# Block attention ahead of two mixtures of experts: the scores and values as 64 by 64 products, q and v sent without zeros, and the first layer's dense products in four banks of PSUM

## What is computed

```python
q_c, k_c, v_c = (a.reshape(B, H, nc, 64, D) for a in (q, k, v))  # B 4, H 8, S 576, D 64
scores = scale * np.matmul(q_c, k_c.transpose(0, 1, 2, 4, 3))    # 64 x 64 for each chunk and head
attn = softmax(scores)                                           # max, exp, sum + 1e-9, divide
x = np.matmul(attn, v_c)                                         # -> (2304, 512), all heads side by side
for e in range(4):   out += p[:, e:e+1] * (relu(x @ w1[e]) @ w2[e])        # first mixture, all rows
for e in range(8):   out[mask] = gate[mask] * (relu(x[mask] @ v1[e]) @ v2[e])  # second, rows of expert e
```

## Time and profile before

| | |
|---|---|
| median of 3 runs | 1189.31 us (1189.1 to 1190.2) |
| time of the profiled execution | 1190.13 us |
| its span | 1188.1 us |
| PE busy | 1172.5 us, 99% of the span |
| weight loads (PEld) busy | 1042.7 us, 88% |
| DVE, ACT, POOL busy | 519.3, 264.5, 312.0 us |
| read from memory | 82.92 MB |

### The profile page before, as it was taken

The page is one execution under the profiler, slowest core; times in us unless marked ns, Lnnn a source line. Parts: engine busy times, 40 slices in busy tenths (PEclk is TensorE's granted clock), DMA queues, the critical chain, the costliest instruction groups (busy, mean ns, idle before and its releaser), DMA issues.

```text
span 1188.1 us, 18269 instructions
## 1 busy us (share of the span) xinstructions
PE 1172.5 (99%) x6211; PEld 1042.7 (88%) x6212; DVE 519.3 (44%) x1142; ACT 264.5 (22%) x413; POOL 312.0 (26%) x191
## 2 busy tenths in 40 slices
PE   9999999999999999999999999999999999999995
PEld 7998998999999999999999999999887888888884
DVE  5542442422222223222222228888745654555554
ACT  3221222223111113211111411211144023022230
POOL 6400000006000003300000600000186868077580
PEclk9999999999999999999999999999999999999998
DMA  9313222042000002100000400111382564063530
GB/s 361 110 66 106 73 86 106 18 143 89 1 0 0 0 0 90 52 0 0 0 0 1 140 1 28 27 27 27 64 267 60 156 190 166 0 207 124 186 143 15
DMA packets 51471, 92.91 MB, mean 78 GB/s; under 512 B 8431, under 2 KB 33135, under 8 KB 51314
## 3 DMA queue, kind: packets, MB, share of 16 engines
q1 hardware_dynamic: 46082, 78.63, 20.6%
q0 software_dynamic: 4496, 11.56, 3.3%
q10 hardware_dynamic: 864, 2.36, 0.5%
HBM read 82.92 MB, written 10.92 MB: 79 GB/s over the span
## 4 chain that ended last, share of the span: by engine, by line
PE 92%; DVE 3%; DMA 2%; ACT 1%; issue 1%; SPq 0%; ACTq 0%; DVEq 0%; POOL 0%; POOLq 0%
PE psum L1245 14%; PE psum L1247 14%; PE psum L1246 14%; PE psum L1276 10%; PE psum L1278 10%; PE psum L1277 10%; PE psum L1455 3%; PE psum L1457 3%; PE psum L1456 3%; PE psum L1187 3%; PE psum L1172 2%; PE psum L1439 2%; DMA rows<-x_rows,meta 1%; PE psum L1416 1%; DVE xlo L759 1%
## 5 line engine op out<-in xcount | busy, mean ns | idle before, releaser
L431 POOL TENSOR_TENSOR weights_r<-weights,weights_r 128x1024 fp32r<-128x1024 f32 x96 | 232.5, 2446 | 652.1 <-ACT weights_r L593 650.9
L1245 PE MATMUL psum<-xhi,weights_r 128*128 128x384 f32 x768 | 259.2, 338 | 1.0 <-DVEq L786 0.4
L1247 PE MATMUL psum<-xhi,weights_r 128*128 128x384 f32 x768 | 256.9, 335 | 0.0
L1246 PE MATMUL psum<-xlo,weights_r 128*128 128x384 f32 x768 | 256.8, 334 | 0.0
L1276 PE MATMUL psum<-weights_r,hhi 128*128 128x512 f32 x576 | 227.3, 395 | 0.0
L1278 PE MATMUL psum<-weights_r,hlo 128*128 128x512 f32 x576 | 224.8, 390 | 0.0
L1277 PE MATMUL psum<-weights_r,hhi 128*128 128x512 f32 x576 | 224.4, 390 | 0.0
L797 DVE SCALAR_TENSOR_TENSOR hlo<-psum,hhi 128x384 fp32r<-128x384 f32 x192 | 106.7, 557 | 217.4 <-ACT hhi L588 217.3
L588 ACT ACTIVATE hhi<-psum 128x384 fp32r<-128x384 f32 x192 | 94.4, 492 | 481.3 <-PE psum L1247 480.7
L1245 PEld LDWEIGHTS psum<-xhi,weights_r 128*128 128x128 f32 x768 | 144.2, 188 | 4.3 <-DVE xlo L759 2.1
L1246 PEld LDWEIGHTS psum<-xlo,weights_r 128*128 128x128 f32 x768 | 144.2, 188 | 0.7
(11 more groups left out here) (185 smaller groups left out, 1165.5 us busy)
## 6 DMA issues: line engine op xcount, KB each, us to landing
weights<-in_moe_w SPq DMA_DIRECT2D x96, 512.0 KB, 5.9
qT<-in_q SPq DMA_DIRECT2D x18, 512.0 KB, 4.3
vbd<-in_v SPq DMA_DIRECT2D x15, 512.0 KB, 3.3
x_rows<-xfin SPq DMA_DIRECT2D x18, 256.0 KB, 4.7
kT<-in_k SPq DMA_DIRECT2D x15, 256.0 KB, 4.4
wg_row<-in_gate_rows SPq DMA_DIRECT2D x1, 2048.0 KB, 7.8
vbd<-in_v ACTq DMA_DIRECT2D x3, 512.0 KB, 9.6
kT<-in_k ACTq DMA_DIRECT2D x3, 256.0 KB, 5.9
```

The source lines that it names most:

```text
L431: gp.tensor_tensor(rounded(set_, 1, c), raw(set_, c), rounded(set_, 0, c).bitcast(F32), ALU.subtract).then_inc(sem("w_lo"), 1)
L1245: mm(out_, ahi, bhi, start=(i == 0), stop=False)
L1246: mm(out_, ahi, blo, start=False, stop=False)
L1247: last = mm(out_, alo, bhi, start=False, stop=(i == n - 1))
```

## The change

- `score` and `attend` become 16 matmuls a tile of 64 by 64 stationary and 64 moving columns. Each takes one quarter of the array: the half of the partitions where its operands lie, and the half of PSUM's partitions where its result goes. `FOURS` runs through the four quarters, so that four in a row use four different ones; the two halves of the contraction side write different banks.
- q and k lie in one array without zeros and come in one transfer of 512 KB a tile; v has no zeros either and comes in 256 KB. All three tiles of a group have buffers of their own for q and k, v, the probabilities and the transposed probabilities.
- The order in a group of the first expert: after step 1 the scores of tiles 0 and 1; after step 5 the scores of tile 2 and the transposes of tiles 0 and 1; after step 8 the values of tiles 0 and 1; after step 10 the transpose of tile 2; after step 12 the values of tile 2.
- The first mixture's dense products use banks 0 to 3: `H_B` is [0, 1, 2, 3, 0, 1, 3, 0] and y lies in banks 1, 2 and 3, for all four experts. Steps 1 to 3 each wait for one tile of y of the group before (formerly step 2 waited for all three), and the first product into the last bank of y waits for the low part of step 6.
- At the start two warm matmuls fewer stand before the scores, one fewer after them, and three are added later; ACT issues its transfers of v after the load of its table.

```diff
-    H_B = [0, 1, 2, 3, 4, 2, 0, 1]
-    Y_B = 2
-    Q_B, K_B, O_B = 5, 6, 7
-    Q0_B, K0_B, O0_B, WARM_B = [5, 0, 1], [6, 2, 3], [7, 5, 7], 4
+    H_B = [0, 1, 2, 3, 0, 1, 3, 0]
+    Y_B = 1
+    S_B = [(4, 5), (6, 7), (5, 6)]
+    PT_B = [4, 7, 4]
+    X_B = [(4, 5), (6, 7), (6, 7)]
+    FIRST_B, FIRST_PT_B, WARM_B = [(4, 5), (6, 7), (2, 3)], 0, 1
...
-    STAGES = {1: [("score", 0)], 4: [("p", 0), ("score", 1)], 7: [("v", 0), ("p", 1), ("score", 2)],
-              10: [("v", 1), ("p", 2)], 13: [("v", 2)]}
...
             for j in range(TG):
-                sp.dma_start(qT[:, j, :, :], q_rows[j * P:(j + 1) * P]).then_inc(qk_in[j], 16)
+                load_qk(j, j)
             for c in range(NW // 2 - 1):
                 load_w(0, w1, w2, 0, c)
-            sp.wait_ge(sem("s_psum"), 1)
-            load_qk(TG, 0)
-            load_v(TG)
+            next_qk(0, 0)
+            next_qk(0, 1)
...
 # DVE
             def attention(step, t0):
-                for stage, j in STAGES.get(step, []):
-                    if stage == "score":
-                        shift(t0 + j)
-                        normalise(t0 + j)
+                if step == 1:
+                    shift(t0, 0, S_B[0])
+                    dve.wait_ge(sem("shifted"), t0 + 1)
+                    shift(t0 + 1, 1, S_B[1])
+                    normalise(t0, 0)
+                if step == 2:
+                    dve.wait_ge(sem("probs_ready"), t0 + 1)
+                    normalise(t0 + 1, 1)
+                if step == 5:
+                    shift(t0 + 2, 2, S_B[2])
+                if step == 6:
+                    normalise(t0 + 2, 2)
...
 # PE
-            def score(t, j, bank=Q_B):
-                for h in range(H):
-                    last = mm(psum[:, bank, h * C:(h + 1) * C], qT[:, j, h, :], kT[:, j, h, :], start=True, stop=True)
+            FOURS = [(0, 0), (1, 1), (0, 1), (1, 0)]
+            def half(i):
+                return slice(i * C, (i + 1) * C)
+            def score(j, banks):
+                for r in range(KT):
+                    for c, odd in FOURS:
+                        last = mm(psum[half(odd), banks[c], r * C:(r + 1) * C], qk_in_tile[half(c), j, 0, 2 * r + odd, :],
+                                  qk_in_tile[half(c), j, 1, 2 * r + odd, :], start=True, stop=True)
                 last.then_inc(sem("s_psum"), 1)
...
-            def attend(t, bank=K_B, v_=vbd[:, :, :, :], p_=pT[:, :, :], rs=range(KT)):
-                pe.wait_ge(sem("pT_ready"), t + 1)
-                for r in rs:
+            def attend(j, banks):
+                for a in range(KP):
                     for c in range(2):
-                        last = mm(psum[:, bank, r * P + c * C:r * P + (c + 1) * C], v_[:, c, r, :],
-                                  p_[:, r, c * C:(c + 1) * C], start=True, stop=True)
+                        for rp, odd in FOURS:
+                            last = mm(psum[half(odd), banks[rp], a * P + c * C:a * P + (c + 1) * C],
+                                      v_tile[half(rp), j, c, a, odd, :], pT[half(rp), j, c * KP + a, half(odd)],
+                                      start=True, stop=True)
+                last.then_inc(sem("o_psum"), 1)
...
             pe.wait_ge(sem("ones_ready"), 1)
-            warm(10)
+            warm(8)
...
+                if 1 <= f <= TG:
+                    pe.wait_ge(sem("y_taken"), n * TG + f)
                 if f == 2:
-                    pe.wait_ge(sem("y_taken"), n * TG + 1)
                     pe.wait_ge(sem("x_ready"), TG)
...
+                    if f == 0 and i == TG - 1:
+                        pe.wait_ge(sem("hlo_ready"), n * FT + FT - 1)
```

More of the change, by code:

```diff
@@ L91, in chunked_attention_then_two_moes @@
     assert a0 + 24576 <= at["acc"]
[L92 to L99, removed]
+    pT = tile("pT", [P, TG, KT, P], F32, at["xfin"])
+    LATE = 12
+    fill = tile("fill", [P, ROWS // P, 2], I32, at["acc"] + 4 * LATE * D)
+    zrow = tile("zrow", [1, D], F32, at["acc"] + 4 * (LATE + 1) * D)
+    assert 8 * (ROWS // P) <= 4 * D and LATE + 2 <= NT
     rows = tile("rows", [P, NB, D], F32, at["acc"])
@@ L151, in chunked_attention_then_two_moes @@
     slot = small("slot", [P, NT], U32)
-    pair = small("pair", [P, NT, 2], I32)
-    pair_f = pair[:, :, :].bitcast(F32)
+    pairs = small("pair", [P, NT, 2], I32)
+    pair_f = pairs[:, :, :].bitcast(F32)
     meta = small("meta", [P, NB + 1, 2], U32)
@@ L214, in chunked_attention_then_two_moes @@
     qk_in = [sem(f"qk_in{i}") for i in range(TG)]
-    v_in = sem("v_in")
-    v_first = [sem(f"v_first{i}") for i in range(TG)]
+    v_in = [sem(f"v_in{i}") for i in range(TG)]
     raw_in = [[sem(f"raw_in{i}_{c}") for c in range(NW)] for i in range(2)]
@@ L314, in _ @@
                 load_w(0, w1, w2, 0, c)
-            sp.wait_ge(sem("s_psum"), TG)
-            load_qk(TG + 2, 2)
-            for j in range(1, TG):
-                next_loads(TG + j, j)
-            with sp.Fori(2, NG - 1) as g:
+            for j in range(TG):
+                next_v(0, j)
+            with sp.Fori(1, NG - 1) as a:
                 for j in range(TG):
-                    next_loads(g * TG + j, j)
-            for j in range(TG):
-                next_loads(NT - TG + j, j, more=(j == 0))
+                    next_qk(a, j)
+                for j in range(TG):
+                    next_v(a, j)
             sp.wait_ge(sem("o_psum"), NT)
@@ L569, in _ @@
[L569 to L571 removed]
+                act.dma_start(v_tile[:, j, :, :, :, :], v_rows[j * P:(j + 1) * P]).then_inc(v_in[j], 16)
             for j in range(TG):
[L573 to L575 removed]
+                exponentials(j, j)
@@ L822, in _ @@
                     attention(f, (g + 1) * TG)
-                for step in range(FT, 2 * FT):
-                    attention(step, (g + 1) * TG)
                 take_xlo(g + 1, g + 1)
@@ L1173, in score, with transpose_p @@
                 last.then_inc(sem("s_psum"), 1)
-            def transpose_p(t, bank=O_B, p=probs[:, :, :]):
+            def transpose_p(t, j, bank):
                 pe.wait_ge(sem("probs_ready"), t + 1)
-                for r in range(KT):
-                    last = tr(psum[:, bank, r * P:(r + 1) * P],
-                              p[:, 2 * r:2 * r + 2, :].rearrange("p h k -> p (h k)"), ident[:, :])
+                p = probs[:, j, :, :, :].rearrange("x c r k -> x (c r k)")
+                for u in range(KT):
+                    last = tr(psum[:, bank, u * P:(u + 1) * P], p[:, u * P:(u + 1) * P], ident[:, :])
@@ L1565 @@
     for name in _INS:
-        a = _laid_out(name, inputs["moe2_w_gate" if name == "gate_rows" else name])
+        if name == "qk":
+            import numpy as np
+            a = np.stack([_laid_out(n, inputs[n]) for n in ("q", "k")], axis=2)
+        else:
+            a = _laid_out(name, inputs["moe2_w_gate" if name == "gate_rows" else name])
         arrays["in_" + name] = a
```

240 lines of the change are left out of this document (131 added, 109 removed).

## The result

The changed kernel takes 1153.97 us (median of 4 runs, 1153.76 to 1154.12), the kernel before 1189.49 us beside it (1189.1 to 1190.2). The ratio is 0.9701, 95% interval 0.9684 to 0.9717: 35.5 us or 3.0% less, where 18 us less were forecast. Its profiled span is 1152.0 us, against 1188.1.

A forecast was written before the change was run, and what follows sets the result against it. PE's issue of its work was taken as the bound. From the profiled 1190.1 us, -14.7 - 2.0 - 2.7 + 1.0 gave 1171.7 us, and 0.8 us off for the median gave 1171 us; range 1150 to 1189 us.

The forecast's parts named there:

- scores and values in the loop, visits included: 30 blocks in five attention groups: each falls from 1.72 to 1.23 us by partly overlapping quarters, -14.7 us.
- wait for xlo: End of each attention group: values of tile 2 one step earlier remove PE's wait in all five groups, -2.0 us.
- start: Before the first dense matmul: earlier q and k and a shorter chain bring it near 20.4 us, -2.7 us (-1 to -4).
- DVE and POOL in group 0: First group: two divisions may both meet POOL's weight subtraction and come late, +1.0 us (0 to 3).
- four banks: Dense products of the first mixture moved to four banks: the tighter waits have cover, so nothing changes.
- four quarters really at once: Rival for scores and values: four quarters run together, 0.6 us a block, about 1151 us; chance 0.13.
- The visits: Entering and leaving the quarters around scores and values: 0.08 us added a block, an estimate.
- No overlap: Rival for scores and values: loads in different quarters follow one another, block stays 1.72 us, about 1188 us; chance 0.13.
- a fixed price: Rival: a 64-column pair costs 107 ns, 3.42 us a block, about 1242 us; chance 0.12, including a costly mode change.
- the threshold of 58 ns: Scores and values: if the pitch of pairs in quarters is above 58 ns, the change loses.
- mostly one wait: Attention group's end: the 0.8 us left beside blocks and transposes was put mostly to PE's wait for xlo.
- they land by 5.5 us: Step of the start: tile 1's q and k, second on their queue, land by 5.5 us.

The follow-up runs named there:

- the two edits: Changed kernel plus 4 and 6 warm matmuls between the start's scores, and row sums of tiles 0 and 1 in PSUM: together 1150.98 us, ratio 0.9676.

## Why the prediction was right in sign and off in size

| term | forecast, us | measured, us |
|---|---|---|
| scores and values in the loop, visits included | -14.7 | -32.5 |
| wait for xlo | -2.0 | -1.4 |
| start | -2.7 | -1.3 and -2.7 in two profiles |
| DVE and POOL in group 0 | +1.0 | -0.4 and +0.8 in the same two |
| four banks | 0 | 0 |

The row on group 0 is what that group takes over the others, 0.10 and 1.35 us, less the 0.52 us that it took over them in the kernel before. The first row is the -34.3 us of the five groups without the -1.4 us of the wait and the -0.4 us of group 0. It agrees with the blocks counted one by one: they took 51.6 us, and 25 slow starts of dense matmuls behind them 25 x 0.087 = 2.2 us more; now scores and values take 5 x (5.64 - 1.3) = 21.7 us, which makes -32.1.

**The blocks: mechanism half right, size wrong. This is the term that was mis-sized.** The prediction put it so: "The two pairs of one float32 product use the same quarter and must follow one another, at about 54 ns; the next product is in another quarter and can begin as soon as issue allows". Both halves hold: 58 ns in one quarter, 7 ns to the next. The error was to add them, product after product, as if PE did not start another quarter's pair until the second pair of this one had begun. In the trace the first pairs of four products start in 20 ns, and 58 ns after the first of them come the second ones. A block is 8 beats x 58.4 = 0.467 us, not 16 x 72 ns = 1.15. No run shows the 15 to 20 ns that the sum took for the next quarter's start. What came true is the rival "four quarters really at once", which had 0.13 and was costed at 0.6 us a block and 1151 us. The argument against it, that no pitch under 40 ns stands in the rows, was drawn from matmuls of the whole array, which can't show this. The Trainium skill, "TensorE: Matmul & The Clock Gate", Part 3, has a few ns for each further tile and was nearer than my sum: the trace has 7 ns where the page says about 4. The Trainium skill, "TensorEngine Tiling (Array Packing)", Instruction Overhead, has about 60 cycles a matmul, by which a block was estimated at 0.8 us; the 0.467 us measured over four quarters do not agree with it. That the point forecast missed by half and the range still held the time is owed to the width of the range, not to the sum.

**The visits: right kind, sized a third.** "For entering and leaving the quarters I add 0.08 us a block", 0.5 us a group. The prediction called itself wrong if the dense matmuls next to a block came late by more than 0.1 us; they came late by about 0.1 us on either side, and more was lost inside the block. Splitting one block in two cost 0.39 us; with four visits a group it is 1.5 us, 7.7 us in the kernel. The prediction also took the 0.08 us from a slow start behind each block of the kernel before, and then charged it to the new blocks alone; the old ones had it too, five times a group, 2.2 us in all. The visits are why joining the blocks of two tiles is worth something: six visits a group would cost 0.8 us more, 3.9 us in all, an estimate from the 0.39 us.

**No overlap and a fixed price** both fall: a pair takes 58.4 ns in one quarter. That is just on the threshold of 58 ns that the prediction gave for a loss, but it is the pitch of one quarter and not of PE: one pair in 14.6 ns is what counts. Even with one quarter at a time the kernel was 0.9% faster than before.

**The wait for xlo** went, as forecast; bringing it back cost 1.4 us, about 0.3 a group where 0.4 was taken. So the 0.8 us a group that the prediction called "mostly one wait" was 0.3 us of wait, and the rest mostly the five slow starts.

**The start** was forecast at 20.4 us for a first dense matmul and came at 21.73 in one profile and 20.36 in the other. The step "they land by 5.5 us" was wrong: q and k of tiles 1 and 2 were used at 6.64 and 8.90 us, as v moved beside them. PE stood idle for it, and the granted clock fell to 0.5 from about 8 to 15 us in the first profile, from about 9 to 12 in the second. That was nowhere in the prediction.

**DVE and POOL in group 0** was right in mechanism ("with 2 us added twice it may come late"), and 1.35 us over the other groups lies in its range of 0 to 3. It missed two things. The kernel before paid 0.5 us for the same cause. And this term and the start are one: with the row sums in SBUF the second division ended at 36.6 us in each of these profiles, so what is gained at the start is lost in group 0. That is why two profiles with starts 1.4 us apart both end group 0 at 60.4 us or 60.5, and why it took the two edits together to bring its end to 58.4.

**Left open:** why the next quarter's pairs begin three pairs early; the look ahead itself is inferred from the spacing and the lengths of the records. Of the 0.4 us by which the stretch behind the attention groups is shorter, 0.34 us lie behind the start of the first mixture's last group. From there the changed kernel's two profiles need 340.33 and 340.25 us to the end, and profiles of versions with the same code there 339.18 to 340.26; the kernel before needs 340.67, and with the new banks alone 340.03. So it is within what profiles differ by.

## What to carry to other kernels

Where small matmuls stand alone on the array, put four independent 64 by 64 ones into the four quarters one after another in program order: the price is then that of the busiest quarter, and a pair of the whole array says nothing about it. Keep such matmuls together, since each excursion from whole-array work has its own price (0.39 us here), and count the excursions before the matmuls. When two engines each bound one stage of a start, an edit for one may show little of its worth alone: look at a fixed point behind both (here the end of group 0), and try them together before either is dropped.

## What the runs showed of the hardware that was not expected

- Float32 pairs of 64 by 64 start every 58 ns in one quarter of the array and 7 ns apart across quarters; 64 of them took 943, 1346 and 2469 ns in fours, twos and ones, for either kind of two.
- Pairs of the next quarter start while three of the quarter before are still to come, by the spacing of the starts and by the eight matmuls of 267 ns among those of 218.
- Going from the whole array to quarters and back costs 0.39 us between dense matmuls.
- A DVE operation on 128x8 numbers, all in SBUF, took 0.17 us without POOL and up to 2.29 us until POOL's subtraction had ended; with its operands in PSUM it kept 0.17 us. The Trainium skill, "SBUF — State Buffer", SBUF: two separate sides, has VectorE and GpSimd share a pair of ports as an exclusive lock; the trace agrees, and shows that an operation can be as small as 8 numbers a partition and still wait for the whole subtraction.
- A PE that was busy for 0.69 of 2 us was followed by a granted clock of 0.5, until 15 us in one profile and 12 us in another of the same kernel; in a third profile with the same start it stayed at 1.00, and so it did with warm matmuls laid in that hole.
